# Attention and two MLP layers: queries split by GpSimd before the transposes, and the first MLP input prepared within the last two heads

## The reference

```
B, H, S, D = 4, 8, 576, 64
scores = q @ k^T / 8 ; causal mask
cum = cumsum(max(s, 0)) ; scores += min(-(cum[i] - cum[j]), 0)
x  = softmax(scores) @ v                      # 32 heads, then x is [4, 576, 512]
xn = (x - mean) / sqrt(var + 1e-6) * g_ln
x  = x + relu(xn @ w1a) @ w2a                 # layer one, 512 -> 2048 -> 512
u  = x + (mixing over tokens by U V, rank 32)
out = u + relu(u @ w1b) @ w2b                 # layer two, same sizes
```

## Time and profile before

| | |
|---|---|
| median of 3 runs | 1116.96 us (1113.01 to 1121.07) |
| the profiled execution, its own time | 1115.07 us |
| its span | 1113.3 us |
| busy: PE, PEld | 1051.2 us (94%), 931.8 us (84%) |
| busy: DVE, ACT, POOL | 811.7 us (73%), 557.2 us (50%), 339.6 us (31%) |

### The profile page before, as it was taken

The page is one execution under the profiler, slowest core; times in us unless marked ns, Lnnn a source line. Parts: engine busy times, 40 slices in busy tenths (PEclk is TensorE's granted clock), DMA queues, the critical chain, the costliest instruction groups (busy, mean ns, idle before and its releaser), DMA issues.

```text
span 1113.3 us, 21040 instructions
## 1 busy us (share of the span) xinstructions
PE 1051.2 (94%) x6936; PEld 931.8 (84%) x6936; DVE 811.7 (73%) x1732; ACT 557.2 (50%) x1265; POOL 339.6 (31%) x377
## 2 busy tenths in 40 slices
PE   6788888888797999999999999999999999999998
PEld 5677777777687898889888889888889888888887
DVE  6899999999558768767767757976865866765532
ACT  5788888888444344444444434443423432433321
POOL 1154453211116433333324232333232423332100
PEclk9999999999898999999999999999999999999999
DMA  5745545445241321322231343432142133223131
GB/s 155 233 120 132 126 120 130 127 119 159 83 134 64 108 76 57 123 68 77 76 114 58 114 151 107 156 112 82 62 138 96 66 100 121 75 84 114 58 127 44
DMA packets 156260, 118.71 MB, mean 107 GB/s; under 512 B 86496, under 2 KB 131552, under 8 KB 156192
## 3 DMA queue, kind: packets, MB, share of 16 engines
q1 hardware_dynamic: 156192, 117.80, 35.2%
HBM read 98.82 MB, written 18.95 MB: 106 GB/s over the span
## 4 chain that ended last, share of the span: by engine, by line
PE 89%; DVE 3%; ACT 3%; issue 2%; DMA 1%; SPq 1%; POOL 0%; ACTq 0%; DVEq 0%; POOLq 0%
PE ps_up L751 9%; PE ps_up L752 9%; PE ps_up L753 9%; PE ps_acc L798 6%; PE ps_acc L797 6%; PE ps_acc L799 6%; PE ps_s L798 5%; PE ps_s L797 5%; PE ps_s L799 5%; PE ps_x L681 5%; PE ps_s L651 3%; PE ps_pt L662 3%; ACT prob L928 2%; PE ps_up L662 2%; PE ps_up L627 2%
## 5 line engine op out<-in xcount | busy, mean ns | idle before, releaser
L751 PE MATMUL ps_up<-z,w 128*128 128x256 f32 x896 | 255.6, 285 | 4.7 <-DVE z L1270 3.8
L752 PE MATMUL ps_up<-z,w 128*128 128x256 f32 x896 | 254.4, 284 | 0.0
L753 PE MATMUL ps_up<-z,w 128*128 128x256 f32 x896 | 254.4, 284 | 0.0
L564 POOL TENSOR_TENSOR w_f<-raw 128x256 f32<-128x256 f32 x64 | 69.0, 1078 | 412.1 <-DMA raw<-in_moe_w_ch 397.4
L751 PEld LDWEIGHTS ps_up<-z,w 128*128 128x128 f32 x896 | 172.3, 192 | 10.6 <-DVE z L1270 4.2
L752 PEld LDWEIGHTS ps_up<-z,w 128*128 128x128 f32 x896 | 172.5, 193 | 5.1
L753 PEld LDWEIGHTS ps_up<-z,w 128*128 128x128 f32 x896 | 172.8, 193 | 0.0
L797 PE MATMUL ps_acc<-w_hi,h 128*128 128x512 f32 x320 | 126.7, 396 | 1.9 <-DVE x_res L1296 1.9
L798 PE MATMUL ps_acc<-w_lo,h 128*128 128x512 f32 x320 | 126.8, 396 | 0.0
L799 PE MATMUL ps_acc<-w_hi,h 128*128 128x512 f32 x320 | 126.2, 394 | 0.0
L1093 ACT ACTIVATE h<-cs 128x768 fp32r<-128x768 f32 x64 | 54.1, 846 | 126.8 <-DVE cs L1383 126.8
(11 more groups left out here) (170 smaller groups left out, 2642.7 us busy)
## 6 DMA issues: line engine op xcount, KB each, us to landing
raw<-in_moe_w_ch SPq DMA_DIRECT2D x80, 512.0 KB, 3.6
ncum_b<-ncum_dram SPq DMA_DIRECT2D x32, 288.0 KB, 3.5
x_in<-x_dram SPq DMA_DIRECT2D x18, 512.0 KB, 4.3
k_raw<-in_k SPq DMA_DIRECT2D x64, 128.0 KB, 2.5
u_dram<-x_in SPq DMA_DIRECT2D x9, 512.0 KB, 2.8
q_raw<-in_q SPq DMA_DIRECT2D x32, 128.0 KB, 3.2
v_raw<-in_v SPq DMA_DIRECT2D x32, 128.0 KB, 2.2
w_f<-in_moe_w_ch SPq DMA_DIRECT2D x4, 1024.0 KB, 8.1
```

The source lines that it names most:

```text
L564: pool.tensor_tensor(to[:, I5, 1], a21, a22, ALU.add).then_inc(s1_done, 1)
L751: nc.tensor.matmul(bank, w_hi, z_hi, start=(start and c == 0), stop=False, skip_group_check=True)
L752: nc.tensor.matmul(bank, w_hi, z_lo, start=False, stop=False, skip_group_check=True)
L753: last = nc.tensor.matmul(bank, w_lo, z_hi, start=False, stop=(stop and c == 1), skip_group_check=True)
```

## The change

GpSimd splits the queries of a head into high and low parts straight from `q_raw`, into a new buffer `q_split` where both parts of 64 lie side by side. PE transposes both at once, 128 columns wide, ACT copies (and scales) all 128 partitions in one instruction, and `q_low` on DVE is gone. `transpose_k` and the scores wait for ACT's copy (`q_done`). `load_q` waits until the head before has been split (`q_lo_done`). On POOL the split of head u + 2 stands ahead of `split_values(u)`; those of heads 0 and 1 stand ahead of the loop.

The first input of layer one is normalised by DVE in head 30 and no longer in head 31. POOL's `inverse_root(0)` stands ahead of `split_values(31)`, ACT scales in head 31 ahead of the exponential of tile 2, PE transposes in two halves (`transpose_first`) within head 31 through the bank `up[0]`, and ACT and DVE split each half (`first_high`, `first_low`) within head 31. `transpose_input(0, 0)`, `z_high(0, 0)` and `z_low(0, 0)` after the last head are gone. Buffers in SBUF are declared in another order.

```
@@ gpsimd
+            def split_queries(u):
+                pool.wait_ge(q_loaded, 16 * u + 16)
+                waits_apart(pool, (qt_done, u))
+                pool.tensor_tensor(q_split[:, :, 0, :], q_raw[:], one[:].unsqueeze(2).to_broadcast([P, QT - 1, D]), ALU.mult).then_inc(q_hi_done, 1)
+                pool.wait_ge(q_hi_done, u + 1)
+                pool.tensor_tensor(q_split[:, :, 1, :], q_raw[:], q_split[:, :, 0, :].bitcast(F32), ALU.subtract).then_inc(q_lo_done, 1)
...
+            split_queries(0)
+            split_queries(1)
             pool.wait_ge(pads_done, 1)
             for u in range(HEADS):
+                if u + 2 < HEADS:
+                    split_queries(u + 2)
+                if u == HEADS - 1:
+                    inverse_root(0)
                 split_values(u)
...
-            inverse_root(0)
@@ sync, load_q
-                wait(sp, qt_done, u)
+                wait(sp, q_lo_done, u)
@@ tensor
-                waits_apart(pe, (q_loaded, 16 * u + 16), (l_lo_done, u))
-                bank = up[0][0:D, :].rearrange("d (n t) -> d t n", t=QT - 1)
+                waits_apart(pe, (q_lo_done, u + 1), (l_lo_done, u))
+                bank = up[0].rearrange("d (n t) -> d t n", t=QT - 1)
                 for t in range(QT - 1):
-                    last = nc.tensor.transpose(bank[:, t], q_raw[:, t], ident)
+                    last = nc.tensor.transpose(bank[:, t], twice(q_split[:, t]).bitcast(F32), ident)
...
-                    pe.wait_ge(q_lo_done, u + 1)
+                    pe.wait_ge(q_done, u + 1)
@@ tensor, head_alone
                 scores(m, p, 3)
+                if final:
+                    transpose_first(0)
                 transpose_probs(m, p, 1)
...
                 transpose_probs(m, p, 2)
+                if final:
+                    transpose_first(1)
...
+            def transpose_first(x):
+                pe.wait_ge(z_done, 2)
+                if x == 0:
+                    pe.wait_ge(l_lo_done, HEADS)
+                else:
+                    pe.wait_ge(first_split, 1)
+                for c in range(2):
+                    for t in range(2):
+                        last = nc.tensor.transpose(up[0][:, c * HT + t * P:c * HT + (t + 1) * P], x_in[:, t, (2 * x + c) * P:(2 * x + c + 1) * P], ident)
+                last.then_inc(*((zt_done, 1) if x else (first_transposed, 1)))
...
-            transpose_input(0, 0, acc)
             times_values(*LAST_HEAD, 0)
@@ scalar
-                nc.scalar.activation(q2s[p][0:D, 0:FULL], up[0][0:D, 0:FULL], ACT.Copy, scale=-SCALE).then_inc(q_hi_done, 1)
+                nc.scalar.activation(q2s[p][:, 0:FULL], up[0][:, 0:FULL], ACT.Copy, scale=-SCALE).then_inc(q_done, 1)
...
                     out_low(*before(m, p), 0)
+                if final:
+                    for t in range(2):
+                        scale_input(0, 0, t)
                 exponential(m, p, 2)
...
                 exponential(m, p, 3)
+                if final:
+                    first_high(0)
...
                 if final:
+                    first_high(1)
                     weights_high(0)
                 probs_high(m, p, 3)
                 exponential(m, p, 4)
-                if final:
-                    for t in range(2):
-                        scale_input(0, 0, t)
...
-            z_high(0, 0, acc)
@@ vector
-            def q_low(m, p):
...
                 probs_low(m, p, 1)
+                if final:
+                    first_low(0)
                 bias_and_max(m, p, 4)
                 if not first:
                     out_sum(*before(m, p), 1)
                 probs_low(m, p, 2)
-                if final:
+                if not more and not final:
                     dve.wait_ge(gain_loaded, 16)
                     normalise(0, 0)
+                if final:
+                    first_low(1)
                     weights_low(0)
-                if more:
-                    q_low(*second(m, p))
...
-            z_low(0, 0, acc)
```

More of the change, by code:

```diff
@@ L156, in chain_kernel @@
             pt_cols = (QT - 1) * ROW + S
+            q2_0, k_hi_0, k_lo_0 = (sbuf(name, [P, n], F32R, small) for name, n in (("q20", SP_PAD), ("k_hi0", S), ("k_lo0", S)))
+            ncum_b = [sbuf("ncum_b0", [P, S], F32, small)]
             pt_his = [sbuf("pt_hi0", [P, pt_cols], F32R, small)]
-            ncum_b = [sbuf(f"ncum_b{p}", [P, S], F32, small) for p in range(2)]
             pt_his.append(sbuf("pt_hi1", [P, pt_cols], F32R, small))
@@ L161, in chain_kernel @@
             prob_2_0 = sbuf("prob_2_0", [P, FULL], F32, small)
-            q2s = [sbuf(f"q2{p}", [P, SP_PAD], F32R, small) for p in range(2)]
             prob_3 = sbuf("prob_3", [P, FULL], F32, small)
@@ L172, in chain_kernel @@
             pt_los = [sbuf("pt_lo0", [P, pt_cols], F32R, small), pt_lo1]
-            k_his = [sbuf(f"k_hi{p}", [P, S], F32R, small) for p in range(2)]
-            k_los = [sbuf(f"k_lo{p}", [P, S], F32R, small) for p in range(2)]
+            q2s, k_his, k_los = ([a, sbuf(name, [P, n], F32R, small)]
+                                 for a, name, n in ((q2_0, "q21", SP_PAD), (k_hi_0, "k_hi1", S), (k_lo_0, "k_lo1", S)))
+            ncum_b.append(sbuf("ncum_b1", [P, S], F32, small))
             prob = [sbuf(f"prob{p}", [P, SP_PAD], F32, small) for p in range(2)]
             q_raw = sbuf("q_raw", [P, QT - 1, D], F32, small)
+            q_split = sbuf("q_split", [P, QT - 1, 2, D], F32R, small)
             k_raw = sbuf("k_raw", [P, QT - 1, 2, D], F32, small)
@@ L231, in chain_kernel @@
         qt_done, kt_done, lt_done = sem("qt_done"), sem("kt_done"), sem("lt_done")
-        q_hi_done, q_lo_done = sem("q_hi_done"), sem("q_lo_done")
+        q_hi_done, q_lo_done, q_done = sem("q_hi_done"), sem("q_lo_done"), sem("q_done")
         k_hi_done, k_lo_done = sem("k_hi_done"), sem("k_lo_done")
@@ L255, in chain_kernel @@
         centred_done, z_done = sem("centred_done"), sem("z_done")
+        first_transposed, first_split = sem("first_transposed"), sem("first_split")
         zt_done, b1_copied, b22_copied = sem("zt_done"), sem("b1_copied"), sem("b22_copied")
@@ L999, in second_high, with first_high @@
                 nc.scalar.activation(w2_hi[:, 2 * j:2 * j + 2], w2_f[:, 2 * j:2 * j + 2], ACT.Copy).then_inc(w2b_hi_done, 1)
+            def first_high(x):
+                act.wait_ge(*((zt_done, 1) if x else (first_transposed, 1)))
+                nc.scalar.activation(z_plain[:, 0, 2 * x:2 * x + 2], up[0].rearrange("p (c r) -> p c r", c=2), ACT.Copy).then_inc(z_hi_a_done, 1)
             def z_high(n, part, banks=zb):
@@ L1256, in second_low, with first_low @@
                                         ALU.subtract).then_inc(w2b_lo_done, 1)
+            def first_low(x):
+                dve.wait_ge(z_hi_a_done, x + 1)
+                nc.vector.tensor_tensor(z_plain[:, 1, 2 * x:2 * x + 2], up[0].rearrange("p (c r) -> p c r", c=2),
+                                        z_plain[:, 0, 2 * x:2 * x + 2].bitcast(F32), ALU.subtract).then_inc(z_lo_a_done if x else first_split, 1)
             def z_low(n, part, banks=zb):
@@ L1342, in prepare @@
                     second_low(j)
-            q_low(0, 0)
             k_low(0, 0)
@@ L1348, in _ @@
                 bias_and_max(0, 0, i)
-            q_low(0, 1)
             k_low(0, 1)
             attention(dve, head_alone)
-            z_low(0, 0, acc)
             invert_sums(*LAST_HEAD)
```

## The result

After: 1135.06 us, the median of four runs (1131.23 to 1137.79); before, in the same session, 1116.84 (1113.01 to 1121.07). The ratio is 1.0154 [1.0119, 1.0189]: slower by 1.2 to 1.9%. The forecast was 1126, with a range to 1134; the loss was foreseen as +10.0 and came out as +18.2. The direction and the mechanism held; the size did not.

The account below looks back on a forecast made before the run. PE's burst plus ACT, not DVE, was taken to bound a head, then the ring of 8.73 us. Steady heads +9.6, start +0.7, end -0.3 made +10.0 on 1115.07: 1125.1, stated as 1126 us, range 1113 to 1134.

Parts of the forecast that it names:

- rival 2: Steady heads: DVE is the bound after all, so each head falls by up to 0.684 us; 1104, full 1095; chance 0.07.
- PE's burst: Steady heads: 6.75 us of gapless PE work plus 1.52 through ACT, together 8.27 a head, with no DVE instruction.
- the ring: Steady heads: value split, SP's query issue, landing, POOL's query split, next value split; 8.73 us a head against PE's 8.46.
- rival 1: Steady heads: queries land sooner, the ring stays hidden and PE's burst decides; 1118.5 us; chance 0.22.
- POOL's two instructions: The query split's mult and subtract on POOL, 128x256 each: 0.70 and 0.73, together taken as 1.42 us.
- rival 3: Steady heads: POOL's query split costs 2.01 us, starts 0.97 apart, so the ring is 9.32; 1140 us; chance 0.06.
- rival 4: Steady heads: landings of 3.5 us and a dearer POOL split, milder, so the ring is 9.03; 1133 us; chance 0.15.
- the start: First heads: POOL's split delays `transpose_q(0)` by 1.5 us, `q_low`'s 0.68 is gone at head 1; net +0.7 (0 to +1.5).
- the steady heads: Heads 3 to 29: PE waits 0.37 us a head at `transpose_q` over 26 turns, +9.6 us.
- the end: Heads 30 and 31 to `up_plain(0)`: +0.9 us from later start, -1.6 if PE keeps 2.4 GHz; taken as -0.3.
- the wider transposes: PE's four query transposes, 128 wide: 0 to +0.15 us a head, taken as +0.08.
- the forecast's case: Steady heads: the ring at about 8.73 us sets the pace and hides the wider transposes; chance 0.50.

Follow-up runs that it names:

- e4: The kernel before with DVE's `q_low` cut to one column, leaving out part of the computation: 1116.42 us, ratio 0.9990.
- e11: The changed kernel without its end part, with SP issuing the queries of head u + 3 ahead of the values of head u + 1: 1116.83 us, ratio 1.0003.
- e3: The changed kernel with SP issuing the queries of head u + 3 ahead of the values of head u + 1: 1118.65 us, ratio 1.0014.
- e5: The changed kernel with POOL's multiply of the query split done twice: 1158.70 us, ratio 1.0381.
- e6: The changed kernel with queries issued early, as in e3, and POOL's multiply of the query split done twice: 1119.34 us, ratio 1.0016.
- e12: The changed kernel with 2 matmuls a head that nobody reads, ahead of `transpose_q` on PE: 1130.36 us, ratio 1.0097.
- e1: The changed kernel without its end part, the first input of layer one prepared after the last head as before: 1130.88 us, ratio 1.0101.
- e9: The kernel before with only the end part moved into heads 30 and 31, plus 26 unread matmuls where PE idles there: 1115.71 us, ratio 0.9990.
- e2: The kernel before with only the first input moved into heads 30 and 31, and the changed buffer order: 1119.24 us, ratio 1.0009.

## Why the prediction came out as it did

**Right: what bounds a head.** DVE at 93% was not the bound: e4 and e11 took load off it for nothing. That refutes rival 2. PE's burst was, and then the ring: opening it (e3) gives the period back, lengthening it (e5) costs in full, lengthening it when open (e6) costs nothing. That refutes rival 1 too.

**Right: the ring's terms.** From value split to issue: 3.94 forecast, 3.92 in the mean of 26 turns. POOL's two instructions: starts 0.69 apart and 0.73 long, forecast 0.70 and 0.73; rival 3 with 0.97 is out. Issue to POOL's start: 3.36 in the mean (3.01 to 3.86), forecast 3.2 and 0.14, so rival 4 did not happen either. POOL's start to the next value split: 1.40 without the waits at the falls, forecast 1.42 and 0.03. The sum of 8.73 stands against 8.67 outside the falls. The Trainium skill's price (DMA: Bandwidth & Descriptors, "Anatomy of one DMA — SWDGE (gpsimd) path"), an estimated 2.3 for these 128 KB, would have hidden the ring; the trace has 3.1 at the median, and the measurement decides. The page gives that price for DMAs that GpSimd issues, and SP issues these. The Trainium skill's rule on the shared port (SBUF — State Buffer, "Who interferes with whom") agrees: from head 3 on, POOL's multiply took 0.612 to 0.654, median 0.614, with DVE busy beside it. Its other half shows at the start, where I did not apply it: beside DVE's scan of two SBUF operands the multiply took 1.36.

**Wrong, the steady heads: the sum had no term for the clock.** I argued that "PE waits at `transpose_q`, 0.37 over today's period" and priced that wait as if PE came back from it at the same pace. The holes (0.36 a head in the weight loads, as forecast), in a stretch that had been at full clock throughout, went with two falls in the profiled execution, 1.45 us each in the ring: 2.9 of the +11.15. e5 bears the price out, e12 does not return it in time. The other three runs have lower clocks (0.982 to 0.986); where their falls lie no trace shows.

**Wrong, the start: "Net +0.7".** It measured +2.45. The price of 1.42 for POOL's pair missed that the first one runs beside DVE's scan (2.16 for the pair, with a multiply of 1.36), and the `q_low` that I set against it at head 1 gave little back: the keys of head 1 still wait, now for ACT's copy of the queries, 1.10 us where it was 1.79. The loss passes through SP's key load and the sums behind it, which I named but gave no price. And some 0.5 of it, the difference to e1, goes with the fall at 22 us.

**Wrong, the end: "Between +0.9 and -1.6: I take -0.3, the middle".** The two ends were the clock lost and the clock kept, and both had it at full speed until `up_plain(0)`. It fell within head 31, at 289, right behind DVE's normalising: ten matmuls of the values took 2.2 rather than 1.3, the transposes of the input 1.11 at half pace, and the start came at 28.7. A third end was missing from the range of that term. e9, which differs from e2 by the clock alone, reached 26.4 and a gain of 1.7, where I had put 1.6. The words "PE, which has no idle piece over 2 us in this plan" were no protection: a piece of 1.43 stood where it fell, and a piece of 2.09 came later.

**Too dear: the wider transposes.** "I take +0.08" and +0.02 for ACT, hidden in the forecast's case but counted in rival 1. Without a wait ahead, the four take 0.60 in e3 and the next matmul starts 0.36 behind their start (205.81 to 206.17), as before with 64 wide (204.94 to 205.30). The true price is 0.

In sum, of the 8.2 us by which the forecast loss was too small, the start is 1.8; the steady heads 1.5 (falls of 2.9, less what the ring outside them was shorter than its sum); the end 2.4; the rest 0.5; and 2.0 lie between the profiled execution (+16.2) and the medians (+18.2), each of four runs that spread by 6.6 and 8.1.

## What to carry to other kernels

Before moving work to an idle engine, write down what stands behind it in that engine's program order, and follow it through the DMA queue to the load that it waits for: a split that took 1.4 us of idle POOL time closed a ring of 8.7 us around a head of 8.36. Where it closes, issue the load earlier, ahead of the wait that the ring runs through; and place what the move has freed where the bounding engine idles, since unloading an engine that is busy for 93% but not in the chain was worth nothing here (e4, e11). Give every hole that a change opens in PE's work a second price, that of the lower clock behind it, with its own branch in the range. And look at what runs on DVE beside each instruction that goes to GpSimd, at the start of the program too.

## What was not expected of the hardware

- GpSimd's multiply beside DVE's scan of two SBUF operands took 1.36 us for a form that takes 0.61 afterwards (1.55 in e12, 1.53 in e1), and ended 0.41 behind the scan in each. It is not that a first instruction is slow: before, GpSimd's first of this kind, at 12.22, took 0.72 like the later ones.
- The clock fell within steady heads to which the change added only PE idle pieces of up to 0.5 us ahead of the query transposes (0.7 in the weight loads), and in two heads of 26, not in every one; with two unread matmuls a head there was none.
- Transposing 64 or 128 columns with the same 128 rows took PE the same time, though the weight load beside it goes from 111 to 141 ns.
- "issue" as the releaser of a wait was twice in after another engine that was late, PE at the lower clock.
